# Fused attention, soft mixture of experts and feed-forward: another order inside the attention step, and weight loads issued earlier

## The reference

```
scores = (q @ k.T) / sqrt(64), plus a distance bias per head, masked outside window and globals
a = exp(scores - max);  a = a / (sum(a) + 1e-9);  attn = a @ v        # 4 batches, 8 heads, 768 x 64
x = attn as tokens (3072 x 512)
logits = x @ phi                                                       # 32 slots
dispatch = softmax of logits over tokens;  slot_input = dispatch.T @ x
slot_out = relu(slot_input @ w1) @ w2, per expert
x = softmax of logits over slots @ slot_out
h = relu(x @ w_in);  out = (h * h) @ w_out
```

## Time and profile before

| | us |
|---|---|
| median of three runs | 519.22 |
| the profiled execution | 519.22 |
| its span | 517.4 |
| batches 1, 2 and 3 of attention, each | 41.80 |
| PE busy over the span | 489.2 (95%) |
| DVE busy | 364.4 (70%) |
| ACT busy | 346.5 (67%) |
| POOL busy | 94.5 (18%) |

### The profile page before, as it was taken

How to read it: one execution, slowest core, us unless ns; L and a number is a source line. 1 busy time by engine, 2 the same in 40 slices (tenths; PEclk the granted TensorE clock), 3 DMA queues, 4 the chain that set the end, 5 groups by cost and what they waited for, 6 DMA issues and landing times.

```text
span 517.4 us, 12778 instructions
## 1 busy us (share of the span) xinstructions
PE 489.2 (95%) x4573; PEld 400.7 (77%) x4573; DVE 364.4 (70%) x1027; ACT 346.5 (67%) x758; POOL 94.5 (18%) x223
## 2 busy tenths in 40 slices
PE   2799999999999998689999999999999999999997
PEld 1566776666766652324689999999999999999996
DVE  5687777777787662404998997687785877868783
ACT  0688887888888720003998986777767777677740
POOL 1455544444544504300000000000000000000000
PEclk9999999999999999699999999999999999999999
DMA  6779889885464599997001010010101101011011
GB/s 240 285 272 326 353 302 327 308 344 209 141 189 161 204 352 395 390 386 293 0 1 41 1 42 10 33 41 0 41 0 41 41 0 41 0 41 41 0 42 41
DMA packets 24587, 77.24 MB, mean 149 GB/s; under 512 B 2528, under 2 KB 2528, under 8 KB 21984
## 3 DMA queue, kind: packets, MB, share of 16 engines
q1 hardware_dynamic: 19680, 60.96, 32.1%
q10 hardware_dynamic: 4864, 15.73, 8.3%
HBM read 70.39 MB, written 6.29 MB: 148 GB/s over the span
## 4 chain that ended last, share of the span: by engine, by line
PE 83%; DVE 6%; ACT 4%; issue 3%; POOL 2%; DMA 1%; ACTq 0%; DVEq 0%; SPq 0%; POOLq 0%
PE bank L1541 14%; PE bank L1540 14%; PE bank L1542 14%; PE bank L1221 7%; PE bank L1209 4%; PE bank L1512 4%; PE bank L1236 4%; ACT probs L965 3%; PE bank L1446 3%; PE bank L1466 3%; PE bank L1241 2%; PE bank L1271 2%; POOL probs L426 2%; PE bank L1261 2%; PE bank L1204 1%
## 5 line engine op out<-in xcount | busy, mean ns | idle before, releaser
L965 ACT ACTIVATE probs<-probs,nmax 128x232 f32<-128x232 f32 (+1 forms) x192 | 88.6, 463 | 37.4 <-DVE nmax L517 37.4
L426 POOL TENSOR_SCALAR probs<-probs,rden 128x232 f32<-128x232 f32 (+1 forms) x192 | 82.5, 448 | 95.9 <-DVE rden L526 95.9
L1540 PE MATMUL bank<-t_hi,s_hi 128*128 128x256 f32 x352 | 98.7, 280 | 0.0
L1541 PE MATMUL bank<-t_lo,s_hi 128*128 128x256 f32 x352 | 98.7, 280 | 0.0
L1542 PE MATMUL bank<-t_hi,s_lo 128*128 128x256 f32 x352 | 98.5, 280 | 0.0
L517 DVE CUSTOM_DVE_ANT_0 probs<-bank,bias 128x232 f32<-128x232 f32 (+1 forms) x192 | 61.8, 378 | 25.5 <-PE bank L1209 22.5
L1088 ACT ACTIVATE g_s<-bank 128x1024 f32<-128x1024 f32 x48 | 49.0, 1022 | 30.6 <-PE bank L1512 30.6
L1117 ACT ACTIVATE s_hi<-s 128x512 fp32r<-128x512 f32 x88 | 55.1, 627 | 19.1 <-DVE s L900 14.6
L1540 PEld LDWEIGHTS bank<-t_hi,s_hi 128*128 128x128 f32 x352 | 66.5, 189 | 0.0
L1541 PEld LDWEIGHTS bank<-t_lo,s_hi 128*128 128x128 f32 x352 | 66.4, 189 | 0.0
L1542 PEld LDWEIGHTS bank<-t_hi,s_lo 128*128 128x128 f32 x352 | 66.4, 189 | 0.0
(11 more groups left out here) (192 smaller groups left out, 999.2 us busy)
## 6 DMA issues: line engine op xcount, KB each, us to landing
qkv_s<-qkv_dram SPq DMA_DIRECT2D x16, 1028.0 KB, 7.7
qkv_s<-qkv_dram SPq DMA_DIRECT2D x16, 704.0 KB, 5.1
w_s<-w_dram ACTq DMA_DIRECT2D x5, 2048.0 KB, 10.5
w_s<-w_dram SPq DMA_DIRECT2D x15, 512.0 KB, 8.6
out_dram<-o_stage SPq DMA_DIRECT2D x24, 256.0 KB, 2.0
w_a<-w_dram SPq DMA_DIRECT2D x9, 512.0 KB, 7.7
wo_raw<-w_out_dram SPq DMA_DIRECT2D x4, 1024.0 KB, 13.1
w_pre<-w_dram ACTq DMA_DIRECT2D x1, 2048.0 KB, 13.0
```

Source lines behind the costliest of these rows:

```text
L426: last = pool.tensor_scalar(probs[:, v % 2, m, a, 0:w], probs[:, v % 2, m, a, 0:w], rden[:, v % 2, m, a:a + 1], 1.0, ALU.mult, ALU.mult)
L965: act.activation(probs[:, v % 2, m, a, 0:w], probs[:, v % 2, m, a, 0:w], ACT.Exp, bias=nmax[:, v % 2, m, a:a + 1], scale=-1.0, accum_out=d ...
L1540: pe.matmul(OUT[n], hi, W_HI[n](at_f), start=(c == 0 and f == 0 and n in (0, 2, 4, 5)), stop=False, skip_group_check=True)
L1541: pe.matmul(OUT[n], hi, W_LO[n](at_f), start=False, stop=False, skip_group_check=True)
```

## The change

On TensorE, `to_tokens` of step s-3 moves from behind the scores to the end of the step, behind the transposes of step s-1. On VectorE, the token copy moves ahead of the bias pass, and takes step s-4 instead of s-3; one more closing step is needed. ScalarE issues six weight loads in steps 1, 3, 5, 7, 9 and 11 of batch 0; the last two of the old list are issued by SyncE, behind the v load of its rounds k = 2 (2 MB) and k = 4 (1 MB).

```diff
@@ SyncE, windowed loads @@
                         load_v(k, n)
+                    if k == 2:
+                        sp.dma_start(w1_c[:, :, :], w1_v[4]).then_inc(w1_c_in, 16)
+                    elif k == 4:
+                        load_win(2)
@@ VectorE step @@
                 def step(b, s, prev):
+                    if s >= 4 or prev:
+                        copy_nat(*before(b, s, 4))
                     if s < STEPS:
                         bias_scores(b, s)
-                    if s >= 3 or prev:
-                        copy_nat(*before(b, s, 3))
                     if (s >= 2 or prev) and s < STEPS + 2:
                         copy_xt(*before(b, s, 2))
...
-                for s in range(STEPS, STEPS + 2):
+                for s in range(STEPS, STEPS + 3):
                     step(LAST, s, True)
@@ ScalarE @@
                 for s in range(STEPS):
                     step(0, s, False)
-                    if s % 4 == 0:
-                        load_early(s // 4)
+                    if s % 2 == 1:
+                        if s < 8:
+                            act.dma_start(w1_s[s // 2][:, :, :], w1_v[s // 2]).then_inc(w1_in[s // 2], 16)
+                        elif s == 9:
+                            act.dma_start(w2_s0[:, :, :], w2_v[0]).then_inc(w2_in[0], 16)
+                        elif s == 11:
+                            act.dma_start(w2_pre[:, :, :], w2_v[1]).then_inc(w2_in[1], 16)
                 for b in range(1, BATCH):
                     for s in range(STEPS):
                         step(b, s, True)
-                        if s % 4 == 0:
-                            load_early((b * STEPS + s) // 4)
@@ TensorE step @@
                 if s < STEPS:
                     scores(b, s)
+                if (s >= 2 or prev) and s < STEPS + 2:
+                    weigh_values(*before(b, s, 2))
+                if (s >= 1 or prev) and s < STEPS + 1:
+                    transpose_probs(*before(b, s, 1))
                 if s >= 3 or prev:
                     if s == 3 and not prev:
                         pe.wait_ge(phi_in, 16)
                     to_tokens(*before(b, s, 3))
-                if (s >= 2 or prev) and s < STEPS + 2:
-                    weigh_values(*before(b, s, 2))
-                if (s >= 1 or prev) and s < STEPS + 1:
-                    transpose_probs(*before(b, s, 1))
```

## The result

The changed kernel takes 530.59 us (530.13 to 531.10, four runs) against 518.78 us (518.02 to 519.45, four runs) for the kernel before in the same comparison: ratio 1.0228, 95% interval 1.0207 to 1.0249. That is 11.8 us slower; 8.8 were forecast, 528.0 us with a range of 521.5 to 532.0. The profiled execution took 530.53 us, its span is 528.8, 11.4 above the 517.4 of before.

A forecast was written before the change was run, and what follows sets the result against it. PE's work set the pace, the latency through POOL 0.2 us behind per three steps. Batch 0 +2.2, batches 1 and 2 +2.5 each, last +2.0, loads 0, behind attention -0.4: +8.8 on 519.22 gives 528.0 us, range 521.5 to 532.

The forecast's parts named there:

- The latency limit: Scores through POOL to scores two steps on: at least 6.50 us before, 6.72 or more with tokens moved in.
- The walk: Score starts of a batch's 12 steps, from PE's step, latency and bias rules: 44.3 us a batch, 41.8 before.
- T(s+2) - T(s): Time on PE from the score start of step s to that two steps on: near 7.3 us for s = 1.
- the written rule: Scores two steps on start at least 5.67 us plus moved work after the bias pass, 5.21 for short tiles.
- The term of the last batch: The last attention batch ends with the latency of its step 11 as before: +2.0 us.
- Batch 0: First attention batch: no dispatch, but mask building stands in the same gap as the copy; +2.2 us.
- The changeover: On PE, tokens behind transposes save one tile-size change, 0.15 us a step, -6.8 us if PE's work set the pace.
- VectorE's copy: Token copy between reciprocals and next bias pass: costs 0 to 0.15 us per step, 0.34 in s = 4 and 5.
- Loads: Reordered weight loads in batches 0 and 1: cost put at 0, with 3 us as upper bound; nothing gained.
- rival 4: A q, k load lands late in batch 1, stall of 1 to 4 us, 530 to 532 us; chance 0.10.
- the sum of bytes on the queue: SP's queue holding 0.7 + 2 + 1 MB at half of 370 GB/s: load lands after some 20 us, 14 available.
- Behind attention: Later stages get some lead for their loads, -0.4 us (0 to -0.75); stages unchanged within 1 us.

The follow-up runs named there:

- e1: The changed kernel with the weight loads of the kernel before, both new orders kept: 527.1 us, ratio 1.0173.
- e6: e1 with two extra identity transposes per step on TensorE, ahead of the wait for POOL's data: 529.7 us, ratio 1.0228.
- e7: e1 with the two token transposes done twice in each step, behind POOL's data: 531.5 us, ratio 1.0263.
- e2: The kernel before with only the weight loads moved, both orders as before: 524.5 us, ratio 1.0123.
- e4: The kernel before with only VectorE's order changed, token copy of step s-4 ahead of the bias pass: 529.1 us, ratio 1.0203.
- e9: e1 with VectorE's token copy of step s-4 behind the bias pass instead of ahead of it: 534.0 us, ratio 1.0301.
- e5: The changed kernel with SyncE's two weight loads two rounds later, at k = 4 and 6: 526.7 us, ratio 1.0160.
- e10: The kernel before with tokens between values and transposes on TensorE in steps 0, 3 and 6 of each batch: 517.1 us, ratio 0.9979.

## Why the prediction was right, and where it was off

*The latency limit: right, within 0.15 us at every step.* The walk gave T = 0, 3.1, 6.4, 10.4, 13.6, 17.0, 21.9, 25.2, 29.3, 32.6, 37.0, 39.8, 44.3 for a batch. Read from score starts of batch 2 after, it is 0, 3.14, 6.41, 10.43, 13.57, 17.00, 21.76, 25.07, 29.17, 32.52, 37.05, 39.83, 44.33. For s = 1, T(s+2) - T(s) was to be near 7.3 and is 7.29. One term of the written rule is a slip: for short tiles 5.21 should be 5.35, which is 6.40 less 1.05; the walk's times come out with 6.40. The term of the last batch was +2.0 and measured +1.9. e1 isolates these terms, and e6 against e7 shows that PE work costs more behind POOL's data than ahead of it.

*Batch 0: near.* +2.2 was forecast for the orders, and e1, which has them alone, measures 2.0. The changed kernel has 1.6: the other 0.4 is won by the loads, since e2, which has those alone, starts batch 1 at 52.55 us rather than 52.99. The prediction had nothing gained by them.

*The changeover: right.* It is gone, by 0.16 us a step, and bought nothing, since PE then waits for POOL.

*VectorE's copy: right in sum, for an incomplete reason.* I priced it by what it delays, the bias pass. e4 and e9 show that its place also decides when tokens may start, a wait that I took as met. In the changed kernel it is met; had I been asked for VectorE's half alone, I would have been wrong by 8 us, as the expectation of e4 was.

*Loads: the mis-sized term.* I took 0 with 3 as upper bound and gave the late q, k load a chance of 0.10 as rival 4. It happened, and the time is that rival's too (530 to 532): the load was issued at 61.81 us and landed after 16.5 us, where some 20 were reckoned and 14 were there. The chain of waits of the changed kernel, PE's timeline behind it and a like step in batch 2, then the issues:

```profile
61.81 16.47 DMA qkv_s<-qkv_dram
78.32 0.80 PE bank L1199 x4
...
78.32 0.80 PE L1199 MATMUL bank<-qkv_s 64*128 64x128 f32 x4 [1.94 <-DMA qkv_s<-qkv_dram]
...
84.37 0.99 PE L1204 MATMUL bank<-qkv_s 64*64 64x168 f32 x16
...
125.15 0.49 PE L1199 MATMUL bank<-qkv_s 64*128 64x128 f32 x4
...
128.46 0.80 PE L1204 MATMUL bank<-qkv_s 64*64 64x168 f32 x16
...
w_c<-w_dram SPq DMA_DIRECT2D x1, 2048.0 KB, 15.6
qkv_s<-qkv_dram SPq DMA_DIRECT2D x1, 1028.0 KB, 16.5
```

It measured +4.5 in batch 1 (48.84 against 44.33), where the sum had 0 and the rival a stall of 1 to 4. The wait itself is 1.94 us. The part missing in the rival is the clock: after the wait the step from 78.32 to 84.37 took 6.05 us at 0.50, the same step of batch 2 takes 3.31, so 2.7 us more. The failure was one of choice: the sum of bytes on the queue, worked out under the rivals, spoke for a stall of 6 us, and I set it aside for a backlog on ScalarE's queue that might end sooner. The half share held: with both queues full, the 704, 2048 and 1028 KB on SyncE's queue took 18.7 us (59.6 to 78.3), about 207 GB/s of some 400.

*Behind attention: -1.6 rather than -0.4*, and not unchanged within 1 us, as the prediction had it. From VectorE's copy `si_t` to the end the profiled execution of before takes 327.0 us, the one after 325.4. Most of it lies in the short stage between the two expert layers, before first:

```profile
208.00:218.00 10.00, 5.69 (x28) 4.50 (x28) 3.83 (x8) 0.00 (x0) 5.17 (x10) 0.63 1.04 388
```

```profile
221.00:229.70 8.70, 4.43 (x28) 3.49 (x28) 3.78 (x8) 0.00 (x0) 5.16 (x10) 0.91 1.04 389
```

The same 28 matmuls ran at a granted clock of 0.63 before and 0.91 after. e1 and e2 also have the shorter stage, e5 the longer one, with the same code there. So it is not the lead of the loads that I had argued for. What decides it from one execution to the next stays open.

With 4.5 for the load in batch 1, -0.6 for batch 0, -0.1 for the last batch and -1.2 behind attention, the forecast's 8.8 becomes the 11.4 of the span. The forecast of 528.0 was thus 2.6 us low by one term, the load, and smaller errors the other way hid a part of it.

## What to carry to other kernels

When work is moved inside an interleaved loop, do not ask only what the busiest engine saves. Write down each loop of dependences that comes round (here scores, exponentials, normalising, transposes, scores two steps on) with its measured length, and see what the moved work had been covering and into which loop it now falls: two limits lay within 0.2 us in three steps of each other here (9.59 and 9.79), a third showed itself once the tokens no longer covered it, and removing PE time helped only in e10, where it was done in three chosen steps of a batch. And when a load is put on a queue, add up the bytes ahead of the next load that somebody needs, at half the bandwidth if another queue is full, and compare with the time until its use.

## What the runs showed of the hardware that was not expected

A wait for a load cost more than itself. In the changed kernel PE waited 1.94 us and the next step took 2.7 us more than a like one; in e2 it waited 4.65 us and the next step took 2.0 us more (77.43 to 82.88, against 121.25 to 124.70 in its batch 2). In both the granted clock behind the wait was 0.50, until about 84.4 and 82.0 us, and 0.98 in the changed kernel over the stretch up to the end of the wait. The shorter wait was not the cheaper one here; each was seen in one profiled execution. Two DMA queues, both full, moved 400 to 413 GB/s together, and the one with the needed load got about half.
